# Tile 0 normalised before it is turned, and q of the first two tiles loaded in whole rows

## What is computed

```
kv_pool = kv.reshape(B, H//4, 4, W//4, 4, C).mean(axis=(2, 4))
k = v = kv_pool.reshape(B, -1, C) @ w_sr
s = (1/sqrt(C)) * (q @ k.T);  s = s - s.max(-1)
a = exp(s);  a /= a.sum(-1) + 1e-9
x = a @ v
h = x @ moe_w_in;   x = (h * sigmoid(1.702 * h)) @ moe_w_out
h = x @ moe2_w_in;  x = (h * clip(h + 3, 0, 6) / 6) @ moe2_w_out
```

## Time and profile before

| | us |
|---|---|
| median of 3 runs | 1321.69 (1320.3 to 1322.43) |
| the profiled execution's own time | 1322.82 |
| its span in the profile | 1321.1 |
| TensorE busy | 1282.8 (97%) |
| VectorE busy | 1042.9 (79%) |
| ScalarE busy | 1034.2 (78%) |
| GpSimd busy | 36.1 (3%) |

### The profile page before, as it was taken

One profiled execution on the slowest core, in us unless ns is written; L12 is line 12 of the kernel. 1 busy time (PEld: TensorE's weight loads), 2 busy tenths in 40 slices (PEclk: granted clock), 3 DMA queues, 4 the chain that ended last, 5 costly groups with the idle time before them and its releaser, 6 DMA issues.

```text
span 1321.1 us, 18302 instructions
## 1 busy us (share of the span) xinstructions
PE 1282.8 (97%) x5748; PEld 1061.3 (80%) x5748; DVE 1042.9 (79%) x1073; ACT 1034.2 (78%) x1211; POOL 36.1 (3%) x43
## 2 busy tenths in 40 slices
PE   6789999999999999999999999999999999999996
PEld 6578888888888888888888888888888888888775
DVE  4778788788888888788888887888888788788666
ACT  2678778788788787887877878878878778788665
POOL 1900000000000000000000000000000000000000
PEclk9999999999999999999999999999999999999999
DMA  8322213113022032130230321312303213112000
GB/s 263 93 62 63 54 19 72 37 35 72 11 61 63 8 72 46 25 72 20 52 70 1 72 48 24 72 29 43 72 2 69 54 17 72 38 26 65 8 0 17
DMA packets 186948, 65.94 MB, mean 50 GB/s; under 512 B 108720, under 2 KB 179504, under 8 KB 186672
## 3 DMA queue, kind: packets, MB, share of 16 engines
q1 hardware_dynamic: 186928, 65.69, 22.1%
HBM read 23.13 MB, written 6.34 MB: 22 GB/s over the span
## 4 chain that ended last, share of the span: by engine, by line
PE 84%; DVE 7%; ACT 5%; issue 2%; DMA 1%; DVEq 0%; ACTq 0%; SPq 0%
PE pair L784 13%; PE pair L786 13%; PE pair L785 13%; PE bank_av L784 8%; PE bank_av L786 8%; PE bank_av L785 8%; PE bank_out L784 7%; PE bank_out L786 6%; PE bank_out L785 6%; DVE mid_lo L662 3%; DVE work L655 3%; ACT mid_hi L459 2%; ACT work L446 2%; PE pair L798 1%; DMA kv_sb<-in_kv_dram 1%
## 5 line engine op out<-in xcount | busy, mean ns | idle before, releaser
L662 DVE TENSOR_TENSOR mid_lo<-work,mid_hi 128x1024 fp32r<-128x1024 f32 (+1 forms) x193 | 235.2, 1219 | 117.9 <-ACT mid_hi L459 117.6
L784 PE MATMUL pair<-x_hi,w_hi 128*128 128x512 f32 x768 | 302.2, 394 | 6.6 <-DVE x_lo L638 5.5
L785 PE MATMUL pair<-x_lo,w_hi 128*128 128x512 f32 x768 | 299.6, 390 | 0.0
L786 PE MATMUL pair<-x_hi,w_lo 128*128 128x512 f32 x768 | 299.5, 390 | 0.0
L646 DVE TENSOR_TENSOR mid_lo<-work,mid_hi 128x1024 fp32r<-128x1024 f32 x192 | 237.4, 1237 | 53.9 <-ACT mid_hi L438 53.9
L431 ACT ACTIVATE work<-pair 128x1024 f32<-128x1024 f32 x192 | 196.9, 1026 | 105.8 <-PE pair L786 105.7
L655 DVE SCALAR_TENSOR_TENSOR work<-work,pair 128x1024 f32<-128x1024 f32 (+1 forms) x193 | 233.1, 1208 | 8.5 <-ACT work L446 8.4
L459 ACT ACTIVATE mid_hi<-work 128x1024 fp32r<-128x1024 f32 (+1 forms) x193 | 202.3, 1049 | 29.5 <-DVE work L655 28.1
L446 ACT ACTIVATE work<-pair,half 128x1024 f32<-128x1024 f32 (+1 forms) x193 | 211.5, 1097 | 11.1 <-PE pair L786 10.4
L438 ACT ACTIVATE mid_hi<-work 128x1024 fp32r<-128x1024 f32 x192 | 202.0, 1052 | 4.9 <-PE bank_av L786 3.4
L784 PEld LDWEIGHTS pair<-x_hi,w_hi 128*128 128x128 f32 x768 | 144.5, 188 | 44.6 <-DVE x_lo L638 6.3
(11 more groups left out here) (87 smaller groups left out, 1506.9 us busy)
## 6 DMA issues: line engine op xcount, KB each, us to landing
p_keys<-p_turned SPq DMA_DIRECT2D x368, 96.0 KB, 2.2
inv_b<-inv_dram SPq DMA_DIRECT2D x24, 256.0 KB, 3.2
q_raw<-in_q_dram SPq DMA_DIRECT2D x92, 64.0 KB, 2.0
out_dram<-y_sb SPq DMA_DIRECT2D x92, 64.0 KB, 2.4
kv_sb<-in_kv_dram SPq DMA_DIRECT2D x7, 768.0 KB, 11.7
w_raw<-in_moe_w_in_dram SPq DMA_DIRECT2D x2, 1024.0 KB, 8.5
inv_dram<-inv_t SPq DMA_DIRECT2D x96, 0.5 KB
kv_sb<-in_kv_dram SPq DMA_DIRECT2D x3, 256.0 KB, 11.7
```

The source lines that it names most:

```text
L662: dve.tensor_tensor(mid_lo[mid2(t, p)][:, part], act2[p % 2][:, part], mid_hi[mid2(t, p)][:, part], ALU.subtract).then_inc(mid2_ready, 1)
L784: pe.matmul(dst, a_hi, b_hi, start=start, stop=False)
L785: pe.matmul(dst, a_hi, b_lo, start=False, stop=False)
L786: return pe.matmul(dst, a_lo, b_hi, start=False, stop=stop)
```

## The change

In SP's queue tile 0's q comes in one transfer of 512-byte rows, the first weight matrix comes right behind it, and tile 1's q follows in four transfers of 512-byte rows. TensorE turns both (`turn_q_first`, 4 transposes each) into `bank_out`, and VectorE's turns go. The second half of the values goes to `bank_out` too.

Tile 0's probabilities are multiplied by their inverse sums on VectorE, slot by slot, before they are turned (`normalise_first`). Then all six chunks are turned in one go into six halves of the three PSUM pairs. `spread_inv(0)`, `inverse(0)` and `scale_x(0)` go; the result of the attention is split straight from PSUM. The scores of tile 1 move behind the turns, and its exponentials behind the split of tile 0's result.

```
-            load_q(0, q_raw, q_loaded)
-            load_q(1, q_raw1, q1_loaded)
-            for n, w in enumerate((w_in1, wo_view[0], w_in2, wo_view[1])):
+            sp.dma_start(q_raw[:, :].rearrange("p (s c) -> p s c", s=SLOTS), q_first).then_inc(q0_loaded, 16)
+            load_weights(0, w_in1)
+            for a in range(4):
+                sp.dma_start(q_raw1[32 * a:32 * (a + 1), :].rearrange("p (s c) -> p s c", s=SLOTS),
+                             q_second[:, a]).then_inc(q1_loaded, 16)
+            load_weights(1, wo_view[0])
...
-            spread_inv(0)
...
+            def turn_q_first(u):
+                if u == 0:
+                    pe.wait_ge(q0_loaded, 16)
+                else:
+                    pe.wait_ge(q1_loaded, 16 * 4)
+                    pe.wait_ge(v_lo_ready, 2)
+                for s in range(SLOTS):
+                    last = pe.transpose(bank_out[:, s * 128:(s + 1) * 128],
+                                        (q_raw, q_raw1)[u][:, s * 128:(s + 1) * 128], ident[:, :])
+                last.then_inc(qt_first_ready, 1)
...
+            def normalise_first(s):
+                part = slice(s, s + 1)
+                dve.wait_ge(exp_ready, s + 1)
+                dve.tensor_scalar(p_sum_eps[:, part], p_sum[:, part], 1e-9, None,
+                                  ALU.add).then_inc(first_sum_ready, 1)
+                dve.wait_ge(first_sum_ready, s + 1)
+                dve.reciprocal(p_inv[:, part], p_sum_eps[:, part]).then_inc(first_inv_ready, 1)
+                dve.wait_ge(first_inv_ready, s + 1)
+                dve.tensor_scalar(slot(probs_first, s), slot(probs_first, s), p_inv[:, part], None,
+                                  ALU.mult).then_inc(first_normed, 1)
...
-                if k > 1:
-                    pe.wait_ge(pt_lo_ready, k - 1)
-                else:
-                    pe.wait_ge(exp_ready, SLOTS)
+                if k == 0:
+                    pe.wait_ge(first_normed, SLOTS)
...
             for s in range(SLOTS):
                 exponential(0, s)
-                if s == 0:
-                    q_high(1)
-            exponential(1, 0)
+            q_high_first(1)
             for k in range(KC):
                 p_hi_first(k)
-                if k % 2 == 1:
-                    exponential(1, 1 + k // 2)
             x1_high(0)
+            for s in range(SLOTS):
+                exponential(1, s)
             load_table(ACT.Gelu_apprx_sigmoid)
```

More of the change, by code:

```diff
@@ L297, in next_q @@
             def next_q(u):
-                hold(qt_ready, u)
+                hold(qt_ready, u - 2)
                 load_q(u, q_raw, q_loaded)
-            spread_inv(0)
             spread_p(1)
@@ L570, in v_lo_part, with q_low_first @@
                 dve.wait_ge(v_hi_ready, h + 1)
-                dve.tensor_tensor(v_lo[:, keys], pair[2][:, h * 512:h * 512 + HALF], v_hi[:, keys],
+                dve.tensor_tensor(v_lo[:, keys], VALUES_IN[h], v_hi[:, keys],
                                   ALU.subtract).then_inc(v_lo_ready, 1)
-            def turn_q(u):
[L575 to L584, removed]
+            def q_low_first(u):
+                dve.wait_ge(q_hi_ready, u + 1)
+                dve.scalar_tensor_tensor(out=(q_lo, q1_lo)[u][:, :], in0=bank_out[:, :], scalar=SCALE,
+                                         in1=(q_hi, q1_hi)[u][:, :], op0=ALU.mult,
+                                         op1=ALU.subtract).then_inc(q_lo_ready, 1)
+            def turn_q(u):
+                dve.wait_ge(q_loaded, 16 * 4 * (u - 1))
+                dve.wait_ge(q_lo_ready, u)
                 dve.transpose(by_slots(q_t), in_blocks(q_raw)).then_inc(qt_ready, 1)
@@ L588, in q_low @@
                 dve.wait_ge(q_hi_ready, u + 1)
-                first = isinstance(u, int) and u == 1
-                full, hi, lo = (q_t1, q1_hi, q1_lo) if first else (q_t, q_hi, q_lo)
-                dve.scalar_tensor_tensor(out=lo[:, :], in0=full[:, :], scalar=SCALE, in1=hi[:, :],
+                dve.scalar_tensor_tensor(out=q_lo[:, :], in0=q_t[:, :], scalar=SCALE, in1=q_hi[:, :],
                                          op0=ALU.mult, op1=ALU.subtract).then_inc(q_lo_ready, 1)
@@ L679, in _ @@
                     v_lo_part(0)
-            turn_q(0)
-            q_low(0)
+            q_low_first(0)
             k_lo_part(1)
             k_lo_part(2)
-            for s in range(SLOTS):
-                maximum(0, s)
-                if s == 0:
-                    v_lo_part(1)
-                    turn_q(1)
-                if s == 2:
-                    q_low(1)
-            maximum(1, 0)
-            inverse(0)
+            maximum(0, 0)
+            v_lo_part(1)
+            maximum(0, 1)
+            maximum(0, 2)
+            normalise_first(0)
+            maximum(0, 3)
+            for s in range(1, SLOTS):
+                normalise_first(s)
+            q_low_first(1)
             for k in range(KC):
                 p_lo_first(k)
-                if k % 2 == 1:
-                    maximum(1, 1 + k // 2)
-            scale_x(0)
+            maximum(1, 0)
+            x1_low(0)
+            for s in range(1, SLOTS):
+                maximum(1, s)
             inverse(1)
-            x1_low(0)
             turn_p(1, 0)
```

135 lines of the change are left out of this document (70 added, 65 removed).

## The result

The changed kernel takes 1324.12 us (median of 22 runs, 1322.37 to 1326.25), the kernel before 1321.99 in the runs beside them (22 runs, 1319.6 to 1323.53): 1.0019 times as long, 95% interval 1.0012 to 1.0026, so 1.6 to 3.4 us more. Two executions beside the experiments, one of the kernel before at a mean clock of 0.85 (1432.93 us) and one of e9 at 0.67 (1802.65 us), are left out of every median and ratio. The profiled execution took 1323.84, its span 1322.1. The forecast was 1324.0.

The account below looks back on a forecast made before the run. TensorE, 97% busy, bounds the kernel; the change moves only when its steady loop begins. First gelu +3.5, first net -1.45, hand-offs +0.25 make +2.3: 1321.7 to 1324.0 us, range 1319.6 to 1328.0.

Parts of the forecast that it names:

- q's turns ahead of the pooling: Prologue, four q transposes on TensorE between the sixth and seventh pooling groups: +0.4 us, first maximum at about 30.7.
- Normalising: VectorE's four slots of tile 0, each waiting for GpSimd's instructions: last multiplication at 42.4 us, against 38.3 undisturbed.
- The rival that the lock doesn't bite: Normalising on VectorE: multiplications find gaps in GpSimd's work, last ends at 38.3, 4.1 us less; total 1319.9; chance 0.18.
- the lock that the prediction describes: VectorE and GpSimd share ports exclusively per whole instruction, taken by two-port modes or two SBUF inputs; no size for itself.
- Turns: TensorE's 24 turns of tile 0's probabilities, 14 at half rate and ten at full: together 3.95 us.
- The first rival: Transposes don't raise the clock: all 24 turns at half rate, 5.0 us, then products too; +2.5, 1326.5 us; chance 0.28.
- Products and scores: Behind the turns, 18 products 4.1 us and two slots of tile 1's scores 2.05; tile 0's attention at 52.65.
- Behind the attention: High part, low part, maxima, tile 1's exponentials and table load: first gelu at 59.2 against 55.71, +3.5 us.
- The first net: Tile 0's first net, GpSimd done at about 60.5: gelu to first product -0.7, first three pairs -0.75, together -1.45 us.
- The rival of late weights: GpSimd starts at 31 as before and meets normalising and first net, losing the 1.45: 1325.4 us; chance 0.05.
- hand-offs: Three new hand-offs between engines of some 0.08 us each: +0.25 us in the sum.
- the list of signs to look for: Expected profile signs: first probability turn at 42 us, gelu at 59, GpSimd done by 61, multiplications 0.8 to 1.9 each.

Follow-up runs that it names:

- e9: Changed kernel with GpSimd held until four slots are normalised, two tile 1 exponentials moved earlier, unread matmuls (22 before the turns, 11 behind between(0)): 0.9994, 1319.66 us.
- e6: Changed kernel with the normalising additions made on two columns instead of one, the second a constant: ratio 1.0037 to the kernel before.
- e3: Changed kernel with GpSimd's first piece of the weights held until tile 0's four slots are normalised: ratio 1.0005 to the kernel before.
- e7: Changed kernel with slots 1 and 3 normalised on ScalarE and the last maximum ahead of slot 0's normalising: ratio 1.0013 to the kernel before.
- e11: Changed kernel with unread matmuls in two places, 32 ahead of the probability turns and 11 behind between(0): ratio 1.0001 to the kernel before.
- e4: Kernel before with unread matmuls, 17 behind tile 0's attention and 11 behind tile 1's attention: ratio 0.9990, 1319.49 us.
- e10: Kernel before with only the change's q part, plus unread matmuls, 17 behind tile 0's attention and 11 behind between(0): ratio 0.9998.
- e8: Changed kernel, slots 1 and 3 normalised on ScalarE, 20 and 11 unread matmuls, two tile 1 exponentials ahead of tile 0's split: ratio 0.9987, 1320.71 us.
- e1: Changed kernel with 32 unread matmuls between tile 0's last scores and the turns of its probabilities: ratio 1.0006 to the kernel before.
- e5: Kernel before with only the change's q part: long rows, first weight matrix right behind tile 0's q, turns on TensorE: ratio 1.0013.

## Why the prediction came out, point by point

The total was right within 0.2 us (1324.12 for 1324.0), and that is luck: errors of up to 2.5 us, of both signs, cancelled. By its own tests ("wrong if the first turn comes before 40 us, or if the gelu comes before 57") it failed: they came at 38.31 and 55.88. 1.6 of that is the earlier start of this execution; counted from the first maximum the tests read +9.3 and +26.3, the turn came at +9.26 and the gelu at +26.83. The timing of the steps is what failed, not the side.

- *q's turns ahead of the pooling*: forecast +0.42, measured +0.39. Right.
- *Normalising*: the step that failed. From the first maximum to the last multiplication 11.7 was forecast, and it took 9.21: 2.5 too dear. "The addition waits for GpSimd's running instruction" came from the 0.87 of a 128x4 addition; on one column it takes 0.14 and doesn't wait, so a slot waits once at most, not twice. e6 gives the second wait back with one more column, and e3 takes the first away. The multiplication alone is 0.62 (0.56 forecast), and all four end 0.41 to 0.44 behind a GpSimd instruction, as the prediction had it (0.42). The rival that the lock doesn't bite had 4.1 us for it and was right in 2.5 of them.
  The Trainium skill has the rule ("VectorE: DVE Perf Modes", section "What auto-detection actually checks"): the two-port mode wants the outermost non-unit dimensions of source and destination both even or equal. The additions and the multiplication have one source, so by the lock that the prediction describes they wait if they are in that mode: 2, 4 and 768 columns do. A single column has no non-unit dimension, and for that the rule is silent; the 0.14 here shows it outside.
- *Turns*: 3.95 forecast, 4.58 measured (38.31 to 42.89). The clock came back 4.2 us after the first turn. In before it was 3.0 after the first product (52.75), at 55.77; the prediction read 2.9 and 55.5 off the end of its window.
  The first rival (only products raise the clock) asked for turns of 5.0 and then products at half rate. The window from 42.5 has 1.00, ahead of the first product at 42.89: it fell. The Trainium skill ("TensorE: Matmul & The Clock Gate", "Part 4: PE-mode transpose") states that rival's rule; this trace and e3's (rise at about 41.7, products from 41.97) speak against it. That transposes count as much as products isn't shown: in e6 and e7 all 24 ran at half clock and the rise came behind the first products.
- *Products and scores*: 6.56 against 6.30 forecast.
- *Behind the attention*: 6.55 forecast to the gelu, 6.43 measured, by the same chain of high part, exponentials and table load.
- *The first net*: -1.45 forecast, -0.45 measured. Gelu to first product went from 4.18 to 3.99 (3.5 forecast), because GpSimd began at 26.84, not 24.7, and ended at 61.77, not 60.5: it still met VectorE's first low part (1.80 for 1.23), and the first three pairs took 8.77, not 8.17.
- *Second fall of the clock*: unforeseen, +1.2 in the profile.

The sum: 2.3 forecast, then -2.5 + 0.6 + 0.3 - 0.1 by the steps ahead of the gelu, +1.0 in the first net, +1.2 at 90, and -0.25 for hand-offs that the measured steps hold already: 2.5. The rival of late weights was right in its kind: part of the 1.45 was lost.

Where the change's cost lies is told by the experiments better than by this list. At equal clock it is 1.9 us (e11 against e4): 0.4 for q's turns ahead of the maximum, and 1.5 behind it, which GpSimd's waits in the normalising (e3) would fill, though the q part isn't ruled out (e10). The rest, 0.6, is that the matmuls nobody reads give the changed kernel a little more back (112.26 - 109.52 = 2.7) than the kernel before (110.15 - 108.00 = 2.15). These are distances of single profiles, good to some tenths.

What the exponentials' place is worth stays open, for it was only tried together with other edits (e8, e9). So does why the clock falls at 90 in some kernels and executions. TensorE waits there for the split of the scaled result, for 2.17 by the timeline, in before, after, e1, e3, e5, e6 and e7; after, e3 and e5 show the fall, the others don't. In the runs beside the experiments the kernel before had the mean clock 0.996 in 40 of 91 (median 1321.67) and 0.998 in 44 (1320.76), though beside e5 to e8 the second group was no quicker (1321.84 against 1321.46); the changed kernel had 0.995 in 17 of 22. So the kernel before has executions with more low clock too, and with the change they are the rule.

## What to carry to other kernels

Before counting a low clock against a change, cure it in the kernel before as well: here matmuls that nobody reads, put into TensorE's gaps, won 1.0 per thousand in the kernel before (e4) and 1.8 in the changed one (e11), about what the whole change lost (1.9). The turns that were gathered into one dense stretch left a gap of 6 us ahead of it, and the stretch began at half rate. And when a price is read from a row of another shape, ask what makes the shape matter: one column instead of four turned a wait into none. A total that comes out proves none of its terms; here the list of signs to look for, and not the total, found the one that was 2.5 us off.

## What the runs showed of the hardware

- VectorE's fp32 addition of 128x1 takes 0.14 while GpSimd's `tensor_tensor` runs; that of 128x2 takes 0.47 to 1.22 (e6), that of 128x4 0.87, and these end as GpSimd's instruction ends.
- fp32 128x768 times a column in SBUF: 0.62 on VectorE alone (e3), 0.74 (e6) to 1.62 (e7) when it waits for one GpSimd instruction; ScalarE's 0.94 (e7).
- 24 turns of fp32 128x128: 2.6 us at 1.00 (e1), 4.98 at 0.50 (e7). The clock rose 3.9 to 4.2 us behind the first turn (e3, after) with no product issued yet, but 5.9 in e7 and 5.4 in e6, when products already ran.
